# Mixing step of a spectral filter in front of a feed-forward network: scaled fp16 parts, moved to the end of odd slots, bias accumulated by TensorE, threshold read from PSUM

## Chip, cores and metric

One core of one Trainium2 chip. The metric is the device time of one execution in microseconds (us); the kernel before has 1456.93 us as the median of 3 runs (1455.4 to 1458.67).

## What is computed

```python
X = np.fft.rfft(x, axis=1)            # x: 4 batches, 3008 tokens, 256 features
Yr = Xr @ w_r - Xi @ w_i + b_r        # the mixing
Yi = Xr @ w_i + Xi @ w_r + b_i
Yr = sign(Yr) * max(abs(Yr) - 0.01, 0)   # the soft threshold, Yi alike
y = np.fft.irfft(Yr + 1j * Yi, n=3008, axis=1)
h = y @ w_in                          # 256 -> 2048
g = (a0 + a1*h + a2*h^2 + a3*h^3) / (1 + |b0|*|h| + |b1|*h^2 + 1e-6)
out = g @ w_out                       # 2048 -> 256
```

## The kernel before

The transform of 3008 = 64 x 47 points is split into matmul stages. **Stage 1** (`step_s1`, 64 groups g, fp32, 96 rows, 512 columns) transforms along 47; its result goes through DRAM. **Stage 2** (`step_s2`, 96 chunks c, 24 to a batch) transforms along 64; ScalarE takes its result out of PSUM into `xt` (`evacuate_s2`, L643, and a negated copy of one half, L644). **Stage 3** (`step_s3`, L438 and L439) is the mixing: four fp32 matmuls of 256 columns with `wr_sb` and `wi_sb` into one bank. VectorE adds the bias and -0.01 (`shifted`, L783, into `t1`), ScalarE makes the lower part of the threshold (`below`, L649), VectorE puts both together (`soft`, L789). **Stage 4** (`step_s4`, L445) is the first half of the inverse transform; `evacuate_s4` (L660) takes it out, and it is stored to DRAM. **Stage 5** (`step_s5`, L468) makes tiles of 470 tokens, which are split into two fp16 parts (L671, L857).

The **network** runs over 26 tiles t in 208 slots q, 8 to a tile. In a slot TensorE issues `group_f2_hi` (L506, L508) and `group_f2_lo` (L521) for slot q-3 and `group_f1` (L491, fp16 parts) for slot q+2. Around them ScalarE has five passes over 128x940 elements (L685, L688, L691, L751, L756), VectorE five (L911, L916, L891, L886, L897), and GpSimd the product `g_lo` (L967), which `group_f2_lo` waits for; a DMA from GpSimd's queue adds `sq` to `den` (L959).

The order of the work is written out by hand. The front (u = 0 to 30) has the first 29 chunks, 32 stage-1 groups, and the splitting of `w_in` and `w_out`. The other 67 chunks go into the slots: stage 2 at the end of an even slot q, stage 3 in slot q+1, stage 4 in slot q+3, both between `group_f2` and `group_f1` (L584 to L606). Stage-1 groups stand at the end of even slots of tiles 0 to 3 and 5 to 8 (`S1_SLOTS`, L114), stage 5 at the end of slots 1 and 3 of each tile 1 to 24 (`S5_AT`, L120). Stages 2, 4 and 5 share the PSUM bank `d0`, stages 1 and 3 the bank `d1`. A stage-5 step waits until every stage-4 result up to its own slot has been taken out of `d0`:

```python
if q and q in S2_AT or q in S5_AT:
    pe.wait_ge(e4, PRE + sum(1 for s in S2_AT if s + 3 <= q))
```

Each engine takes its instructions in order. ScalarE in iteration q: stage-2, stage-1 and stage-5 evacuations of slot q-1, `group(q+1)` with `below` inside it, a finished tile's output (L744, in slot 2 of a tile), L751 of q, `evacuate_s4`, L756 of q. VectorE in iteration q: L911, `shifted`, L916 of q, the stage-5 split, L891 of q-2, L886 of q-1, `soft`, L897 of q-2. `group_f1(q+2)` waits for L916 of q. GpSimd: L967 after L897, then L959. SyncE's queue issues all loads and stores of the transform.

Of the kernel before, what the change touches and what calls it, by code (L numbers as in the profile page):

```python
# [7 lines left out]
F32 = mybir.dt.float32  # L8
# [115 lines left out]
W_AT = 16  # L124
ENTRY = [t for t in range(2, NT) if len(tile_parts(t)) == 2]
# [40 lines left out]

def done_by(table, q, before):
    return before + sum(1 for s in table if s <= q)


def spectral_ffn(nc, x, c1, c5, fwd, inv, w_r, w_i, bias, w_in, w_out, coef_a, coef_b, out):
    with ExitStack() as ctx:
# [17 lines left out]
        wr_sb, wi_sb = sb("wr_sb", P, KH, D), sb("wi_sb", P, KH, D)  # L190
# [13 lines left out]
        qone, lam2 = sb("qone", P, 1), sb("lam2", P, 1)  # L204
# [8 lines left out]
        xt = several("xt", 2, P, KH, 192)  # L213
        t1, neg = sb("t1", P, D), sb("neg", P, D)
# [37 lines left out]
        STAGE = num + sq  # L252

# [26 lines left out]
        def _(sp):  # L280
# [137 lines left out]
        def _(pe):  # L418
# [16 lines left out]
            def step_s3(c, bank):  # L435
                pe.wait_ge(e2, (c + 1) * 2)
                for h in range(KH):
                    pe.matmul(bank[:, 0:D], xt[c % 2][:, h, 64:192], wr_sb[:, h, :], start=h == 0, stop=False)  # L438
                    mm = pe.matmul(bank[:, 0:D], xt[c % 2][:, h, 0:128], wi_sb[:, h, :], start=False, stop=h == 1)  # L439
                mm.then_inc(p3, 1)  # L440

            def step_s4(c, bank):
                pe.wait_ge(s_inv[c % 4], (c // 4 + 1) * 16)
                pe.wait_ge(m_thr, c + 1)
                pe.matmul(bank[:, 0:D], inv_in[c % 4][:, :], ythr[c % 2][:, :], start=True, stop=True).then_inc(p4, 1)  # L445

# [551 lines left out]
```

## Time and profile before

| | us |
|---|---|
| median of 3 runs | 1456.93 |
| the profiled execution, its own time | 1455.9 |
| its span in the profile | 1454.0 |
| TensorE matmul busy | 1411.5 (97%) |
| VectorE busy | 1261.2 (87%) |
| ScalarE busy | 1223.1 (84%) |
| GpSimd busy | 631.7 (43%) |

Busy shares are means over stages. Matmuls overlap in the records: the time that one takes is read from the start of one to the start of the next, or from the chain, which cuts them that way. An fp32 matmul has two records. The same holds on ScalarE and VectorE, where a record begins some 0.1 us before the one ahead of it has ended.

### The profile page before, as it was taken

How to read it: one execution, taken by the hardware profiler on the slowest of the kernel's cores; microseconds unless marked ns; L12 is line 12 of the kernel's file. 1: busy time of each engine (PE TensorE's matmuls, PEld its weight loads, DVE VectorE, ACT ScalarE, POOL GpSimd, SP SyncE). 2: the span in 40 equal slices, each digit the busy share in tenths (PEclk: the TensorE clock that was granted, in tenths of full speed). 3: DMA queues.
4: the chain of work that ended last, by engine and by line, in shares of the span. 5: the costliest groups of instructions: out<-in, count | busy, mean ns of one | idle time of the engine just before them, and what ended most of it. 6: DMA issues, size and time to landing. Idle time of an engine off the chain costs nothing.

```text
span 1454.0 us, 20392 instructions
## 1 busy us (share of the span) xinstructions
PE 1411.5 (97%) x7008; PEld 1004.7 (69%) x7008; DVE 1261.2 (87%) x1466; ACT 1223.1 (84%) x1687; POOL 631.7 (43%) x417
## 2 busy tenths in 40 slices
PE   7998999999999999999999999999999999999987
PEld 2886777777777777777777777776766666666666
DVE  0355988988988889889899989989989999999998
ACT  3567888988988888889878888888988999999986
POOL 0000444444444444445445545444545555555554
PEclk9999999999999999999999999999999999999999
DMA  9875666566466655655555555555554555555443
GB/s 276 246 249 140 144 156 135 134 143 145 100 138 140 144 117 130 142 103 124 110 120 112 122 110 118 120 110 106 116 115 100 100 105 111 115 113 105 89 96 70
DMA packets 97845, 188.00 MB, mean 129 GB/s; under 512 B 11152, under 2 KB 57680, under 8 KB 97744
## 3 DMA queue, kind: packets, MB, share of 16 engines
q0 software_dynamic: 29952, 98.58, 37.1%
q1 hardware_dynamic: 67792, 88.12, 20.6%
q8 instruction: 58, 0.95, 0.3%
q14 instruction: 43, 0.35, 0.1%
HBM read 50.60 MB, written 37.49 MB: 61 GB/s over the span
## 4 chain that ended last, share of the span: by engine, by line
PE 70%; DVE 17%; issue 5%; ACT 5%; DMA 2%; POOL 1%; SPq 0%; ACTq 0%; DVEq 0%; POOLq 0%
PE h_ps L491 23%; PE o_ps L521 8%; PE o_ps L506 8%; PE o_ps L508 8%; DVE den L891 4%; DVE num L897 4%; DVE g_hi L886 4%; PE d L439 4%; PE d L438 4%; DVE num L911 4%; PE d L468 3%; PE d L445 3%; PE d L431 2%; PE d L425 2%; PE h_ps L438 2%
## 5 line engine op out<-in xcount | busy, mean ns | idle before, releaser
L967 POOL TENSOR_TENSOR g_lo<-num,sq 128x940 fp32r<-128x940 f32 (+1 forms) x205 | 457.4, 2231 | 127.4 <-DVE num L897 127.2
L959 POOL DMA_DIRECT2D den<-sq x208 | 182.8, 879 | 682.4 <-PE o_ps L521 380.3
L506 PE MATMUL o_ps<-g_hi,wout_hi 128*128 128x470 f32 (+1 forms) x832 | 345.0, 415 | 0.9 <-DVE g_hi L886 0.9
L508 PE MATMUL o_ps<-g_hi,wout_lo 128*128 128x470 f32 (+1 forms) x832 | 310.3, 374 | 0.0
L491 PE MATMUL h_ps<-yt_hi,win_hi 128*128 128x470 f16 (+1 forms) x832 | 301.5, 362 | 3.9 <-DVE num L916 3.9
L491 PE MATMUL h_ps<-yt_lo,win_hi 128*128 128x470 f16 (+1 forms) x832 | 300.0, 361 | 0.0
L491 PE MATMUL h_ps<-yt_hi,win_lo 128*128 128x470 f16 (+1 forms) x832 | 299.6, 360 | 0.0
L685 ACT ACTIVATE den<-h_ps,coef 128x940 f32<-128x940 f32 (+1 forms) x208 | 214.2, 1030 | 53.1 <-PE h_ps L491 49.8
L916 DVE SCALAR_TENSOR_TENSOR num<-num,coef,h_ps 128x940 f32<-128x940 f32 (+1 forms) x208 | 244.5, 1175 | 5.0
L521 PE MATMUL o_ps<-g_lo,wout_hi 128*128 128x470 f32 (+1 forms) x832 | 225.9, 393 | 21.4 <-POOL g_lo L967 20.7
L897 DVE SCALAR_TENSOR_TENSOR num<-num,a_sb,den 128x940 f32<-128x940 f32 (+1 forms) x208 | 244.8, 1177 | 0.1
L886 DVE SCALAR_TENSOR_TENSOR g_hi<-num,a_sb,sq 128x940 fp32r<-128x940 f32 (+1 forms) x208 | 244.6, 1176 | 0.0
L911 DVE TENSOR_TENSOR num<-h_ps,num 128x940 f32<-128x940 f32 (+1 forms) x208 | 232.0, 1116 | 11.2 <-ACT num L691 11.0
L891 DVE SCALAR_TENSOR_TENSOR den<-den,g_hi 128x940 f32<-128x940 f32 (+1 forms) x208 | 237.1, 1140 | 0.1
L691 ACT ACTIVATE num<-h_ps,coef 128x940 f32<-128x940 f32 (+1 forms) x208 | 234.2, 1126 | 0.0
L688 ACT ACTIVATE sq<-h_ps,coef 128x940 f32<-128x940 f32 (+1 forms) x208 | 215.0, 1034 | 22.2 <-POOL g_lo L967 21.7
L751 ACT ACTIVATE sq<-den,qone 128x940 f32<-128x940 f32 (+1 forms) x208 | 223.4, 1074 | 3.2 <-DMA den<-sq 3.0
L756 ACT ACTIVATE sq<-sq 128x940 f32<-128x940 f32 (+1 forms) x208 | 204.2, 982 | 4.5
L521 PEld LDWEIGHTS o_ps<-g_lo,wout_hi 128*128 128x128 f32 x832 | 151.2, 189 | 58.8 <-POOL g_lo L967 40.4
L506 PEld LDWEIGHTS o_ps<-g_hi,wout_hi 128*128 128x128 f32 x832 | 158.0, 190 | 33.9 <-issue 8.3
L508 PEld LDWEIGHTS o_ps<-g_hi,wout_lo 128*128 128x128 f32 x832 | 158.1, 190 | 23.5 <-issue 7.4
L491 PEld LDWEIGHTS h_ps<-yt_hi,win_hi 128*128 128x128 f16 x832 | 81.4, 98 | 99.9 <-issue 33.3
(101 smaller groups left out, 1405.0 us busy)
## 6 DMA issues: line engine op xcount, KB each, us to landing
den<-sq POOLq DMA_DIRECT2D x200, 470.0 KB, 4.4
spec<-s1w SPq DMA_DIRECT2D x64, 192.0 KB, 3.2
z_in<-spec SPq DMA_DIRECT2D x96, 128.0 KB, 3.3
spec<-s_out SPq DMA_DIRECT2D x96, 128.0 KB, 3.3
xw<-in_x SPq DMA_DIRECT2D x31, 384.0 KB, 4.5
out_t<-o_sb SPq DMA_DIRECT2D x25, 470.0 KB, 4.7
zp_in<-spec SPq DMA_DIRECT2D x22, 480.0 KB, 4.8
inv_in<-in_inv SPq DMA_DIRECT2D x96, 64.0 KB, 2.4
```

What stands on the lines that cost most here:

```text
L491: mm = pe.matmul(h_ps[q % 2][:, j, 0:cols(q)], w[:, h, f * P:(f + 1) * P], y[t % 2][:, h, 0:cols(q)], start=i == 0, stop=i == len(terms) - 1)
L506: pe.matmul(o_ps[:, h, 0:w], wout_hi[:, f, h * P:(h + 1) * P], g_hi[q % 3][:, j, 0:w], start=f == 0, stop=False)
L508: mm = pe.matmul(o_ps[:, h, 0:w], wout_lo[:, f, h * P:(h + 1) * P], g_hi[q % 3][:, j, 0:w], start=False, stop=False)
L521: mm = pe.matmul(o_ps[:, h, 0:w], wout_hi[:, f, h * P:(h + 1) * P], g_lo[q % 2][:, j, 0:w], start=False, stop=f == FB - 1)
L691: act.activation(ring(num, q), h, ACT.Identity, bias=scales(q // SLOTS, 4), scale=scales(q // SLOTS, 5)).then_inc(n_num, 1)
L751: act.activation(ring(sq, q), ring(den, q), ACT.Abs_reciprocal_sqrt, bias=qone[:, 0:1]).then_inc(n_rs, 1)
L886: dve.scalar_tensor_tensor(out=g_hi[r % 3][:, :, 0:w], in0=ring(num, r), scalar=a_sb[:, 0:1], in1=ring(sq, r), op0=ALU.add, op1=ALU.mult). ...
L891: dve.scalar_tensor_tensor(out=ring(den, r), in0=ring(den, r), scalar=1.0 + 1e-6, in1=g_hi[r % 3][:, :, 0:cols(r)].bitcast(F32), op0=ALU.a ...
L897: dve.scalar_tensor_tensor(out=ring(num, r), in0=ring(num, r), scalar=a_sb[:, 0:1], in1=ring(den, r), op0=ALU.add, op1=ALU.subtract).then_ ...
L911: dve.tensor_tensor(top, h, top, ALU.mult).then_inc(n_n2, 1)
L916: dve.scalar_tensor_tensor(out=top, in0=top, scalar=scales(q // SLOTS, 1), in1=h, op0=ALU.add, op1=ALU.mult).then_inc(n_n3, 1)
L967: pool.tensor_tensor(g_lo[r % 2][:, :, 0:cols(r)], ring(num, r), ring(sq, r), ALU.mult).then_inc(n_g, 1)
```

## The change

It stores `w_r` and `w_i` as two scaled fp16 parts each (scale from their largest value), measures every batch of `x` by the sums of its absolute values, and scales the stage-2 result by that into fp16: ScalarE writes the upper part, VectorE the lower part and the negated halves. The mixing becomes one matmul that puts bias times scale into the bank and twelve fp16 matmuls. `shifted` and `t1` go; `below` and `soft` read the bank. The scale is taken out in `evacuate_s4`. Stages 4 and 3 move behind `group_f1`, `evacuate_s4` behind L756. The loads of `w_r`, `w_i` and the bias move up in SyncE's queue, into the stage-1 loop.

```diff
 # SyncE
             def load_x(k):
                 if k >= 4:
                     sp.wait_ge(p1, 2 * (k - 3))
+                    if k - 3 <= FRONT_S1 // 2:
+                        sp.wait_ge(x_dve, 2 * (k - 3))
+                    else:
+                        sp.wait_ge(x_act, 2 * (k - 3) - FRONT_S1)
...
+                if g == 8:
+                    load(mix_stage(0), w_r.rearrange("(h p) e -> p h e", p=P), s_wc)
+                    load(mix_stage(1), w_i.rearrange("(h p) e -> p h e", p=P), s_wc)
+                    load(bias_sb[:, :], bias, s_wc)
             load_fwd(0)
-            load(wr_sb[:, :, :], w_r.rearrange("(h p) e -> p h e", p=P), s_wc)
-            load(wi_sb[:, :, :], w_i.rearrange("(h p) e -> p h e", p=P), s_wc)
-            load(bias_sb[:, :], bias, s_wc)
 # TensorE
             def step_s3(c, bank):
-                pe.wait_ge(e2, (c + 1) * 2)
+                upper, lower = xt[c % 2][:, 0], xt[c % 2][:, 1]
+                pe.wait_ge(k_bias, 6)
+                pe.wait_ge(k_x, X_STEPS * (c // K2 + 1))
+                pe.matmul(bank[:, 0:D], picks[c // K2][:, :], bias_rows[:, :], start=True, stop=False)
+                pe.wait_ge(e2l, c + 1)
                 for h in range(KH):
-                    pe.matmul(bank[:, 0:D], xt[c % 2][:, h, 64:192], wr_sb[:, h, :], start=h == 0, stop=False)
-                    mm = pe.matmul(bank[:, 0:D], xt[c % 2][:, h, 0:128], wi_sb[:, h, :], start=False, stop=h == 1)
+                    pe.matmul(bank[:, 0:D], upper[:, h, 64:192], wr_hi[:, h, :], start=False, stop=False)
+                    pe.matmul(bank[:, 0:D], upper[:, h, 64:192], wr_lo[:, h, :], start=False, stop=False)
+                    pe.matmul(bank[:, 0:D], lower[:, h, 64:192], wr_hi[:, h, :], start=False, stop=False)
+                pe.wait_ge(e2n, c + 1)
+                for h in range(KH):
+                    pe.matmul(bank[:, 0:D], upper[:, h, 0:128], wi_hi[:, h, :], start=False, stop=False)
+                    pe.matmul(bank[:, 0:D], upper[:, h, 0:128], wi_lo[:, h, :], start=False, stop=False)
+                    mm = pe.matmul(bank[:, 0:D], lower[:, h, 0:128], wi_hi[:, h, :], start=False, stop=h == KH - 1)
                 mm.then_inc(p3, 1)
...
                 for r in done:
                     group_f2_hi(r)
-                if q - 3 in S2_AT:
-                    step_s4(c, d0[:, :])
                 for r in done:
                     if r < NS - 2:
                         group_f2_lo(r)
+                if q + 2 < NS:
+                    group_f1(q + 2)
+                if q - 3 in S2_AT:
+                    step_s4(c, d0[:, :])
                 if q - 1 in S2_AT:
-                    pe.wait_ge(m_t, c)
+                    pe.wait_ge(m_thr, c)
                     step_s3(c, d1[:, :])
-                if q + 2 < NS:
-                    group_f1(q + 2)
 # ScalarE
-                act.activation(xt[c % 2][:, :, 64:192], both, ACT.Copy).then_inc(e2, 1)
-                act.activation(xt[c % 2][:, :, 0:64], both[:, :, 64:128], ACT.Copy, scale=-1.0).then_inc(e2, 1)
+                act.wait_ge(k_x, X_STEPS * (c // K2 + 1))
+                act.activation(xt[c % 2][:, 0, :, 64:192], both, ACT.Identity,
+                               scale=x_scale[:, c // K2:c // K2 + 1]).then_inc(e2, 1)
+            def sum_abs(g):
+                act.activation(x_size[0:ROWS, :], x_in[...], ACT.Abs,
+                               accum_out=x_sum[0:ROWS, g:g + 1]).then_inc(x_act, 1)
...
                     act.activation(ring(sq, q), ring(den, q), ACT.Abs_reciprocal_sqrt, bias=qone[:, 0:1]).then_inc(n_rs, 1)
-                if q - 3 in S2_AT:
-                    evacuate_s4(S2_AT[q - 3], d0[:, :])
                 if q < NS:
                     act.wait_ge(n_rs, q + 1)
                     act.activation(ring(sq, q), ring(sq, q), ACT.Square).then_inc(n_rec, 1)
+                if q - 3 in S2_AT:
+                    evacuate_s4(S2_AT[q - 3], d0[:, :])
+                if q in S1_AT:
+                    sum_abs(S1_AT[q])
 # VectorE
+            def lower_x(c, bank):
+                dve.wait_ge(e2, c + 1)
+                dve.scalar_tensor_tensor(out=xt[c % 2][:, 1, :, 64:192], in0=both, scalar=x_scale[...],
+                                         in1=xt[c % 2][:, 0, :, 64:192], op0=ALU.mult, op1=ALU.subtract).then_inc(e2l, 1)
+                dve.wait_ge(e2l, c + 1)
+                dve.tensor_scalar(xt[c % 2][:, :, :, 0:64], xt[c % 2][:, :, :, 128:192], -1.0, None, ALU.mult).then_inc(e2n, 1)
...
-                if q - 2 in S2_AT:
-                    shifted(S2_AT[q - 2], d1[:, :])
                 if q < NS:
                     (L916)
+                if q - 1 in S2_AT and q >= 2:
+                    lower_x(S2_AT[q - 1], d0[:, :])
```

Added besides, in words: `sum_abs` of the 32 stage-1 groups of the front on VectorE (a `tensor_reduce` of 96x512 elements, one per group); at the start on VectorE the bias rows, the largest of `w_r` and `w_i`, six small steps for their scale and two subtractions for their lower parts, on ScalarE their upper parts; `measure_x(n)`, nine small dependent VectorE steps for each batch n, at the start, at u = 20, and in iterations 34 and 76, each behind a small matmul of TensorE (`sum_x`). The first stage-2 evacuation waits for `measure_x(0)`.

## Rows read from the trace of the kernel before

**Rows 1.** Busy time by stretch (busy us and count per engine, clock, DMA share, GB/s).
```profile
34.00:126.00 92.00, 91.80 (x459) 75.62 (x460) 41.83 (x118) 53.52 (x164) 0.00 (x0) 0.99 0.77 232
146.00:400.00 254.00, 253.72 (x1261) 183.88 (x1259) 224.06 (x249) 219.20 (x308) 114.64 (x75) 1.00 0.62 137
...
700.00:1000.00 300.00, 298.06 (x1512) 216.88 (x1513) 277.80 (x323) 260.85 (x353) 141.76 (x92) 1.00 0.55 117
1000.00:1300.00 300.00, 290.16 (x1440) 197.19 (x1438) 290.03 (x294) 271.12 (x308) 156.32 (x102) 0.99 0.53 108
```

**Rows 2.** Chain that ended last, slots 1 to 5 of a tile without stage 1 (start, us, what).
```profile
863.64 1.09 PE d L468 x10
...
869.71 0.44 PE d L431 x4
...
871.89 0.43 PE d L445 x2
872.32 0.94 PE o_ps L521 x4
873.26 0.43 PE d L438 x2
873.70 0.43 PE d L439 x2
...
874.99 2.38 PE h_ps L491 x12
```

**Rows 3.** Groups by line and shape, TensorE.
```profile
L508 PE MATMUL o_ps<-g_hi,wout_lo 128*128 128x470 f32 x800 | 300.6, 376 | 0.0
L491 PEld LDWEIGHTS h_ps<-yt_lo,win_hi 128*128 128x128 f16 x832 | 82.0, 99 | 69.5 <-issue 1.0
L438 PEld LDWEIGHTS d<-wr_sb,xt 128*128 128x128 f32 x268 | 50.8, 190 | 7.0
```

**Rows 4.** Groups by line and shape, ScalarE and VectorE.
```profile
L649 ACT ACTIVATE neg<-t,lam 128x256 f32<-128x256 f32 x96 | 48.6, 506 | 3.8 <-DVE t L783 3.8
L783 DVE TENSOR_TENSOR t<-d,bias_sb 128x256 f32<-128x256 f32 x67 | 27.9, 417 | 1.2
L643 ACT ACTIVATE xt<-d 128x256 f32<-128x256 f32 x67 | 25.2, 376 | 0.0
L644 ACT ACTIVATE xt<-d 128x128 f32<-128x128 f32 x67 | 18.2, 272 | 0.0
L636 ACT ACTIVATE s1w<-d 96x512 f32<-96x512 f32 x32 | 19.0, 595 | 4.9 <-PE d L425 4.9
L795 DVE TENSOR_REDUCE w_top<-num 128x1 f32<-128x1024 f32 x4 | 4.8, 1209 | 0.0
L698 ACT ACTIVATE win_hi<-num,w_scale 128x1024 f16<-128x1024 f32 x4 | 4.5, 1134 | 0.0
L700 ACT ACTIVATE wout_hi<-sq 128x1024 fp32r<-128x1024 f32 x4 | 4.2, 1045 | 0.0
L834 DVE TENSOR_SCALAR coef<-y_rec 128x1 f32<-128x1 f32 x7 | 1.1, 154 | 0.2
L865 DVE TENSOR_SCALAR minus_one<-ident 128x128 f16<-128x128 f32 x1 | 0.2, 217 | 0.0
```

**Rows 5.** Timeline of ScalarE, slots 2 and 3 of a tile with stage 1.
```profile
534.81 0.99 ACT L756 ACTIVATE sq<-sq 128x940 f32<-128x940 f32 x1
535.70 0.36 ACT L643 ACTIVATE xt<-d 128x256 f32<-128x256 f32 x1
...
540.71 1.00 ACT L756 ACTIVATE sq<-sq 128x940 f32<-128x940 f32 x1
543.46 0.65 ACT L671 ACTIVATE yt_hi<-d,coef 128x470 f16<-128x470 f32 x1 [1.75 <-PE d L468]
```

**Rows 6.** Timelines of GpSimd and VectorE, slots 4 and 5 of the tile of rows 2.
```profile
869.86 2.22 POOL L967 TENSOR_TENSOR g_lo<-num,sq 128x940 fp32r<-128x940 f32 x1 [1.14 <-DVE num L897]
...
870.85 1.19 DVE L916 SCALAR_TENSOR_TENSOR num<-num,coef,h_ps 128x940 f32<-128x940 f32 x1
```

**Rows 7.** Timeline of the start.
```profile
25.32 0.45 SPq L282 DMA_DIRECT2D wr_sb<-in_w_r  x1
...
31.40 0.29 DVE L777 TENSOR_SCALAR bias_sb<-bias_sb 128x256 f32<-128x256 f32 x1 [24.90 <-DMA bias_sb<-in_bias]
...
33.09 0.38 ACT L643 ACTIVATE xt<-h_ps 128x256 f32<-128x256 f32 x1 [4.38 <-PE h_ps L431]
```

More of the change, by code:

```diff
@@ L659, in evacuate_s4 @@
                     act.wait_ge(s_st4[c % 2], c // 2 * 16)
-                act.activation(s4_out[c % 2][:, :], bank[:, 0:D], ACT.Copy).then_inc(e4, 1)
+                act.activation(s4_out[c % 2][:, :], bank[:, 0:D], ACT.Identity,
+                               scale=x_inv[:, c // K2:c // K2 + 1]).then_inc(e4, 1)
             def evacuate_s5(idx, bank):
@@ L776, in _ @@
+            for g in range(FIRST_SUMS):
+                sum_abs(g)
             dve.wait_ge(s_wc, 16 * 3)
             dve.tensor_scalar(bias_sb[:, :], bias_sb[:, :], LAM, None, ALU.subtract).then_inc(k_dve, 1)
-            dve.wait_ge(k_dve, 9)
-            def shifted(c, bank):
-                dve.wait_ge(p3, c + 1)
-                dve.wait_ge(m_thr, c)
-                dve.tensor_tensor(t1[:, :], bank[:, 0:D], bias_sb[:, :], ALU.add).then_inc(m_t, 1)
-            def soft(c):
+            dve.wait_ge(k_dve, 8)
@@ new lines, in _ @@
+            dve.tensor_scalar(bias_rows[:, :], bias_sb[:, :], 1.0, None, ALU.mult).then_inc(k_bias, 1)
+            dve.memset(pick[:, :], 0.0).then_inc(k_bias, 1)
+            dve.wait_ge(k_bias, 2)
+            for half in range(2):
+                lo = half * 64 + 32
+                dve.scalar_tensor_tensor(out=bias_rows[lo:lo + 32, :], in0=bias_sb[lo:lo + 32, :], scalar=1.0,
+                                         in1=bias_rows[lo:lo + 32, :].bitcast(F32),
+                                         op0=ALU.mult, op1=ALU.subtract).then_inc(k_bias, 1)
+                dve.memset(pick[half * 64:half * 64 + 64, half * 64:half * 64 + 64], 1.0 / 32).then_inc(k_bias, 1)
@@ new lines, in _, with measure_x @@
+            dve.wait_ge(k_mix, 6)
+            for g in range(FIRST_SUMS, S1N + 4):
+                sum_abs(g)
+            def measure_x(n, part):
+                one, before = slice(n, n + 1), X_STEPS * n
+                dve.wait_ge(x_tot, n + 1)
+                dve.tensor_reduce(x_top[:, one], part, mybir.AxisListType.X, ALU.add).then_inc(k_x, 1)
+                dve.wait_ge(k_x, before + 1)
+                dve.tensor_scalar(x_top[:, one], x_top[:, one], 2.0 ** -50, None, ALU.max).then_inc(k_x, 1)
+                dve.wait_ge(k_x, before + 2)
+                dve.tensor_scalar(x_binade[:, one].bitcast(I32), x_top[:, one].bitcast(I32), 0x7F800000, None,
+                                  ALU.bitwise_and).then_inc(k_x, 1)
+                dve.wait_ge(k_x, before + 3)
+                dve.reciprocal(x_rec[:, one], x_binade[:, one]).then_inc(k_x, 1)
+                dve.tensor_scalar(x_inv[:, one], x_binade[:, one], 2.0 ** -3, mix_k[:, 0:1], ALU.mult, ALU.mult).then_inc(k_x, 1)
+                dve.wait_ge(k_x, before + 4)
+                dve.tensor_scalar(x_scale[:, one], x_rec[:, one], 2.0 ** 3, None, ALU.mult).then_inc(k_x, 1)
+                dve.tensor_scalar(x_out[:, one], x_rec[:, one], 2.0 ** 3, mix_scale[:, 0:1], ALU.mult, ALU.mult).then_inc(k_x, 1)
+                dve.wait_ge(k_x, before + 7)
+                dve.tensor_scalar(x_lam[:, one], x_out[:, one], -2.0 * LAM, None, ALU.mult).then_inc(k_x, 1)
+                dve.tensor_scalar(picks[n][:, :], pick[:, :], x_out[:, one], None, ALU.mult).then_inc(k_x, 1)
+                dve.wait_ge(k_x, before + X_STEPS)
@@ L859, in split_lo @@
                                          op0=ALU.mult, op1=ALU.subtract).then_inc(e5l, 1)
+            for i, (part_hi, part_lo) in enumerate(((wr_hi, wr_lo), (wi_hi, wi_lo))):
+                dve.wait_ge(mix_hi, i + 1)
+                dve.scalar_tensor_tensor(out=part_lo[:, :, :], in0=mix_stage(i), scalar=mix_scale[:, 0:1],
+                                         in1=part_hi[:, :, :], op0=ALU.mult, op1=ALU.subtract).then_inc(mix_lo, 1)
+            measure_x(0, d1[:, 0:S1N])
+            lower_x(0, h_ps[0][:, 0, :])
             for u in range(1, PRE + 1):
-                shifted(u - 1, h_ps[1][:, (u - 1) % 2, :])
+                if u < PRE:
+                    lower_x(u, h_ps[0][:, u % 2, :])
                 if u == W_AT + 11:
```

165 lines of the change are left out of this document (130 added, 35 removed).

## The prediction
> **What bounds the kernel now.** I read the busy times by stretch first, then the chain, then the timelines around the moved steps. In the front (34 to 126 us) and in the slots with spectral work (146 to about 1000) TensorE has next to no idle time: 91.80 of 92.00, 253.72 of 254.00 and 298.06 of 300.00 us [rows 1]. Behind it VectorE is at 224 of 254 and 278 of 300, ScalarE at 219 and 261. From 1000 on VectorE is the full one (290.03 of 300) with TensorE at 290.16; there the 96 mixing steps are nearly all done. So columns taken from TensorE are time up to about 1000 us, as long as the order of the work doesn't turn them into waits.
>
> **The mixing on TensorE.** Today: four fp32 matmuls, 0.43 us apart and 1.73 in all (873.26 to 874.99) [rows 2]. After: twelve fp16 matmuls of 256 columns. A record of stage 2 is also 256 column cycles (128 columns, two passes), and four of them take 0.44, 0.11 each [rows 2]; a stretch of twelve with 470 fp16 columns takes 2.38, 0.198 each, 0.42 ns per column, so 256 give 0.108. Twelve are 1.30. The bias matmul by L508's pace (0.214 for 470, eight in the 1.73 of a group) is 0.12. Sum 1.42, saving 0.31 a step: 67 x 0.31 = 20.8 us in the slots and 29 x 0.31 = 9.0 in the front, **29.8 together**. Bounds for one step: 1.35 below, 1.6 above (a change between number formats costs up to 0.1, twice).
> Whether the weight loads stay hidden decides this. An fp16 load has a record of 99 ns, an fp32 load 190 [rows 3], and stage 2 hides the longer one behind the same 256 cycles, so I take them as hidden. The Trainium skill, TensorE: Matmul & The Clock Gate, The mechanism, says that a load overlaps matmuls in flight only when its row group differs, which here it never does. By that rule a pair would take 0.108 + 0.099 = 0.21, a step 2.6 us, and the sum would be 80 us slower instead. By that rule the 2.38 us of twelve fp16 matmuls would be impossible too, so the trace speaks against it.
>
> **VectorE.** Out goes L783 (0.42, net 0.34), in come the lower part (by L783's form about 0.4) and the negation of 256 fp16 elements (by L865's 217 ns for 128, and at most 0.4) [rows 4]: +0.3 a chunk, four chunks a tile, 1.2 us on a tile's 53 to 56 us, against the 7 to 12% that it is idle [rows 1]. It stays covered as long as TensorE bounds; over the last 20 chunks, where VectorE is at 93% and more, it may cost up to 3 us, 0 taken. The lower part waits for the stage-2 evacuation, which ends about 536.1 [rows 5], some 5 us ahead of stage 3's new place. The Trainium skill, SBUF — State Buffer, Who interferes with whom, says that a `tensor_scalar` in a two-port mode and a GpSimd operation lock each other out for a whole instruction. By it the negation could wait for `g_lo`. `g_lo` ends at 872.08, L916 in front of the lower part at about 871.96 [rows 6], so the lower part passes the remainder and the sum would not change by more than 0.2 us a chunk in front of an engine with slack.
>
> **ScalarE.** L644 goes (net 0.15), an Identity with a scale costs 0.09 over a Copy (L698 against L700), twice, and each stage-1 group in the slots gets `sum_abs`: L636's 0.59 + 0.13 (L649's accumulating form against L643's) + 0.09 to read the sum - 0.1 overlap = 0.7 [rows 4]. `below` waits for stage 3 itself, no longer for VectorE: it comes 1.9 us behind `group_f1`, just what two passes ahead of it take, so 0.
>
> **What the new order turns into waits.**
> (a) Stage 5 in slot 3 needs the stage-4 result of its own slot out of the bank. Today that result came before `group_f1`; now 1.4 us before stage 5, and its evacuation stands behind L756. With stage 1 in the tile: L756 starts at 540.71 [rows 5]; -0.15 + 0.09 + 0.70 ahead of it, -0.27 for the evacuation that leaves, +0.13 for the semaphore that it covered, gives 541.21, +0.89 for the pass, +0.36 for the evacuation, +0.1: stage 5 can start at 542.55. TensorE would be there at 543.46 - 0.20 - 1.09 - 0.31 = 541.86. Loss 0.7 in 7 tiles: **4.9**. In the 10 tiles without stage 1 ScalarE is 1.2 earlier and TensorE 0.85: nothing left to wait for.
> (b) `group_f2_lo` loses stage 4's cover. In slot 5 GpSimd ends at 872.08 [rows 6], the group begins at 872.32 + (0.94 - 0.86) = 872.40 [rows 2], and would now be due at 871.89: 0.5 of wait against 0.08 today. Loss 0.43 in the 10 tiles without stage 1 (with it, 0.85 us more lie ahead): **4.3**. Slot 1 of these tiles is half as tight: **2.0** (0 to 4.3).
> (c) `measure_x` of two batches in iterations 34 and 76 stands in front of L897, nine dependent steps at L834's 0.154 and more, 1.5 us, and by `g_lo` it reaches `group_f2_lo`: **3.0** (0 to 4).
> (d) Front: where the network's weights are split (8 of 29 steps) ScalarE's round (0.36 + 0.49 + 0.36 + 1.05 and waits) is as long as TensorE's new 2.3, and `measure_x(1)` falls there; the DMA share is already 0.77: **3.5** of the 9.0 (1 to 8).
> (e) Start: today L643 begins at 33.09, and the weights' loads are issued at 25.3 behind the stores [rows 7]. They move to about 15 us, three issues of 0.45 and 640 KB in front of stores; on VectorE follow bias rows (2 us), two maxima (0.65 each by L795), eight sums of stage-1 input (0.65), two lower parts (0.65), `measure_x(0)` 1.7; I get the first stage-2 evacuation at about 35 instead of 33.1, and add the stores' delay: **3.0** (0 to 7).
> The moved stage 4 makes its store some 4 us later; what is queued behind it on SyncE (z, inverse matrices, stage-1 stores, the next tile's input) is issued more than a slot ahead of its use, the tightest at the batch borders in slots 39 and 87. Taken as 0; if the slack is gone, 2 to 4 us at two places. `shifted`'s place, the renumbered waits at the start and `lower_x` at q = 0 cost nothing: TensorE has `group_f1(0)` over them.
>
> **Sum.** 29.8 - 4.9 - 4.3 - 2.0 - 3.0 - 3.5 - 3.0 = 9.1 us less than the profiled execution's 1455.9, 1446.8; the median of the runs is 1.0 above that execution, so **1448**.
>
> **Rivals.**
> A, the columns come through nearly whole: the waits (a) and (b) are covered by slack that I don't see, since ScalarE begins its passes 1.9 us earlier relative to the slot's end. For it: 1.75 us of idle ScalarE before L671 [rows 5]. Against it: that idle time is counted in (a). Time: 1457 - 29.8 + 6 = 1433; chance 0.16.
> B, slower: in the slots with stage 5 ScalarE becomes the bound. Its place is the wait on `e4` in front of L468, its price 1 us a tile for each us that ScalarE gets later, in all 17 tiles with chunks. It decides from 0.6 us beyond my sum on (9.1 over 17). `sum_abs` or the fp16 evacuation priced too low, or L751 waiting for its DMA once ScalarE runs earlier, would do it; at 1.2 us beyond it 20 us are lost: 1459, at 1.5 some 1464. For it: VectorE and GpSimd hang on the same iterations. Against: every pass has its row. Chance 0.14.
> C, weight loads not hidden (above), 1535: 0.02.
> D, the gain is spent in full but no more: start and front at their upper bounds (7 and 8): 1456.5, 0.10.
> E, the change doesn't do what it says, as the pace of an fp16 matmul with 256 columns is 0.13: nothing is saved, 1457 + 6 = 1463, 0.04.
> My forecast (gain of 3 to 16) has 0.54.
>
> **Numbers.** What a measurement can tell from no change is about 0.2%, 2.9 us. Faster by more: 0.54 + 0.16 = 0.70 (all of forecast and A), within 0.12, slower 0.18 (B, C, E and the upper end of D). The range reaches from 1434 (A) to 1461 (most of B, all of D); outside are C and E, the far end of A and of B.
>
> **What would show it.** Stage-3 steps of 1.4 us in the chain, twelve records 0.108 apart; waits of some 0.7 us in front of L468 in slot 3 of tiles with stage 1, released by the stage-4 evacuation; waits for `g_lo` in odd slots; TensorE idle some 2% in 146 to 1000 where it had none; a tile with stage 1 shorter by about 0.5 us. Wrong would be: a pace over 0.12; the stage-5 wait over 1 us in all tiles; a front that is no shorter; or stretches from 1000 on that change.

## The result, and the profile after

The changed kernel takes 1453.92 us (median of 20 runs, 1451.39 to 1456.76), the kernel before, run beside it, 1457.84 (20 runs). The ratio of the two is 0.9977, 95% interval 0.997 to 0.9984: **3.9 us by the medians, 0.23% by the ratio, faster**. That is inside the range (1434 to 1461), with 3.9 us gained where 9 were forecast. The profiled execution has a span of 1451.9 us against 1454.0.

The head of the page of the changed kernel (busy us, share, count):

```profile
span 1451.9 us, 21569 instructions
...
PE 1394.3 (96%) x7498; PEld 972.0 (67%) x7498; DVE 1319.5 (91%) x1645; ACT 1253.8 (86%) x1657; POOL 630.4 (43%) x417
```

TensorE's busy time fell by 17 us, the span by 2. VectorE's rose by 58 (some of it the sums of `x` in the front). The stretches, to be laid beside [rows 1]:

```profile
34.00:126.00 92.00, 88.90 (x632) 71.73 (x632) 57.87 (x172) 58.31 (x142) 0.30 (x1) 0.99 0.79 236
146.00:400.00 254.00, 250.72 (x1362) 177.05 (x1361) 231.03 (x287) 230.18 (x317) 114.01 (x75) 1.00 0.62 138
400.00:700.00 300.00, 294.86 (x1600) 207.38 (x1599) 272.59 (x334) 268.37 (x368) 132.89 (x88) 1.00 0.57 127
700.00:1000.00 300.00, 294.87 (x1614) 208.37 (x1612) 283.89 (x343) 264.11 (x331) 141.37 (x92) 0.99 0.54 117
```

TensorE now has gaps everywhere: 3.3 us of 254, 5.1 of 300 and 5.1 of 300, where it had 0.3, 0.5 and 1.9. The mixing step in the chain (start, us, what), to be laid beside [rows 2]:

```profile
858.92 0.43 PE d L486 x2
859.36 0.12 PE d L470
859.47 0.12 PE d L473
859.60 0.11 PE d L474
...
860.69 0.11 PE d L480
860.80 1.10 PE d L522 x10
```

From 859.36 to 860.80 it takes 1.44 us, where it took 1.73. That is what was predicted for the mixing; the loss is elsewhere. The new and changed instructions by form (busy us, mean ns, idle before and its releaser), against [rows 3, 4]:

```profile
L743 ACT ACTIVATE s_out<-d,x_inv 128x256 f32<-128x256 f32 x96 | 45.0, 468 | 11.1 <-PE d L486 5.0 <-DMA spec<-s_out 3.9 <-PE d L511 1.2
L931 DVE SCALAR_TENSOR_TENSOR xt<-d,x_scale,xt 128x256 f16<-128x256 f32 x67 | 32.2, 480 | 10.7 <-ACT xt L715 10.7
L934 DVE TENSOR_SCALAR xt<-xt 128x256 f16<-128x256 f16 x96 | 21.8, 227 | 3.3
L723 ACT ACTIVATE x_size<-xw 96x512 f32<-96x512 f32 x32 | 19.7, 615 | 0.0
L475 PEld LDWEIGHTS d<-wr_hi,xt 128*128 128x128 f16 x134 | 13.1, 98 | 1.5
```

And who keeps TensorE waiting between 146 and 1000 us (waits: us in total, times, longest):

```profile
PEld o_ps L575 <- POOL g_lo L1134: 17.6, 22, 2.5
PE o_ps L575 <- POOL g_lo L1134: 9.9, 18, 2.1
PEld d L522 <- ACT s_out L743: 6.1, 8, 1.0
PE d L522 <- ACT s_out L743: 3.8, 8, 0.6
```

L575 is `group_f2_lo`, L522 stage 5. These are the two waits (a) and (b) of the prediction. (The waits of PE and of its weight loads PEld overlap and are not to be added.) Of the 9.9 us in front of L575, 5.5 are three waits that (b) does not have: 1.65 and 1.70 behind the two measurements, 2.12 at a batch border.

**Tile by tile.** The loop was measured tile by tile, from the start of VectorE's first pass (L911, now L1073) in one tile's first slot to that in the next tile's. Length of a tile in us:

| tile (first slot) | before | after | change | predicted |
|---|---|---|---|---|
| stage 1, four chunks (16, 24, 48, 56, 64; mean) | 55.79 | 55.42 | -0.37 | -0.54 |
| the same, batch border (40) | 55.82 | 56.25 | +0.43 | -0.54 |
| four chunks, `measure_x` (32, 72; mean) | 53.51 | 55.17 | +1.66 | +0.9 |
| four chunks (80, 104, 120; mean) | 52.94 | 52.26 | -0.68 | -0.6 |
| four chunks, batch border (88) | 54.40 | 56.14 | +1.74 | -0.6 |
| three chunks (96, 112, 128; mean) | 50.60 | 51.13 | +0.53 | -0.3 |

(The predicted column divides the prediction's own terms: 0.31 a chunk, less 0.7, less 0.43 + 0.2, or plus 1.5.) Two tiles of the loop are not in the table: tile 8 went from 55.79 to 55.64, tile 136, the last with mixing steps, from 55.94 to 54.06. From slot 8 to slot 144 all adds up to 918.5 us before and 919.7 after. All that the kernel gained it gained ahead of slot 8 (4.4 us there, 3.2 at slot 144, 2.0 at slot 152 and from there on); tiles 136 and 144 together have -0.7 (-1.88 and +1.21).

### The profile page after: what moved, and what is told of

The parts are those of the page before. It is cut to its first block, busy times and chain, and to the rows that moved or that the text cites. A ratio compares the mean times of both kernels' runs of the same rounds, so it can differ in the third digit from the quotient of the medians.

```text
span 1451.9 us, 21569 instructions
## 1 busy us (share of the span) xinstructions
PE 1394.3 (96%) x7498; PEld 972.0 (67%) x7498; DVE 1319.5 (91%) x1645; ACT 1253.8 (86%) x1657; POOL 630.4 (43%) x417
## 3 DMA queue, kind: packets, MB, share of 16 engines
HBM read 50.60 MB, written 37.49 MB: 61 GB/s over the span
## 4 chain that ended last, share of the span: by engine, by line
PE 53%; DVE 22%; ACT 11%; issue 7%; POOL 4%; DMA 2%; SPq 0%; ACTq 0%; DVEq 0%; POOLq 0%
PE h_ps L545 18%; PE o_ps L575 7%; DVE den L1053 5%; DVE num L1059 5%; PE o_ps L560 5%; DVE g_hi L1048 5%; PE o_ps L562 5%; POOL g_lo L1134 4%; DVE num L1073 3%; PE d L522 3%; PE d L486 2%; ACT num L775 2%; ACT sq L772 2%; ACT den L769 2%; ACT sq L839 2%
## 5 line engine op out<-in xcount | busy, mean ns | idle before, releaser
L1134 POOL TENSOR_TENSOR g_lo<-num,sq 128x940 fp32r<-128x940 f32 (+1 forms) x205 | 452.1, 2205 | 176.6 <-DVE num L1059 176.0
L560 PE MATMUL o_ps<-g_hi,wout_hi 128*128 128x470 f32 (+1 forms) x832 | 341.1, 411 | 2.2 <-DVE g_hi L1048 2.2
L575 PE MATMUL o_ps<-g_lo,wout_hi 128*128 128x470 f32 (+1 forms) x832 | 216.7, 382 | 31.4 <-POOL g_lo L1134 30.7
L1073 DVE TENSOR_TENSOR num<-h_ps,num 128x940 f32<-128x940 f32 (+1 forms) x208 | 231.8, 1115 | 8.1 <-ACT num L775 7.8
L839 ACT ACTIVATE sq<-den,qone 128x940 f32<-128x940 f32 (+1 forms) x208 | 223.4, 1074 | 3.3 <-DMA den<-sq 3.3
L575 PEld LDWEIGHTS o_ps<-g_lo,wout_hi 128*128 128x128 f32 x832 | 150.6, 189 | 74.0 <-POOL g_lo L1134 55.7
```

The costliest lines, as they stand in the source:

```text
L560: pe.matmul(o_ps[:, h, 0:w], wout_hi[:, f, h * P:(h + 1) * P], g_hi[q % 3][:, j, 0:w], start=f == 0, stop=False)
L575: mm = pe.matmul(o_ps[:, h, 0:w], wout_hi[:, f, h * P:(h + 1) * P], g_lo[q % 2][:, j, 0:w], start=False, stop=f == FB - 1)
L839: act.activation(ring(sq, q), ring(den, q), ACT.Abs_reciprocal_sqrt, bias=qone[:, 0:1]).then_inc(n_rs, 1)
L1073: dve.tensor_tensor(top, h, top, ALU.mult).then_inc(n_n2, 1)
L1134: pool.tensor_tensor(g_lo[r % 2][:, :, 0:cols(r)], ring(num, r), ring(sq, r), ALU.mult).then_inc(n_g, 1)
```

## The experiments

All times are medians beside runs of the kernel before on the same chip (1456.9 to 1457.6 there). Tiles are named by their first slot. The diffs are against the changed kernel, except for the first.

Two limits hold for all of them. The changed kernel was not run again beside them, and the kernel before moved by up to 0.9 us between the sets (1456.94 to 1457.84), so a difference from the changed kernel is good to about 1 us. And one execution of each kernel is profiled: its first stage-2 matmul begins at 33.56 us in the changed kernel and at 33.89 to 36.24 in its variants, also where the edit is only in the slots. So what an edit does in the slots is read from the lengths of the tiles, and the medians say it only roughly.

### The new order alone

The order of the change in the kernel before, arithmetic as it was (TensorE's part is shown; the stage-4 evacuation also goes behind L756):

```diff
+                if q + 2 < NS:
+                    group_f1(q + 2)
                 if q - 3 in S2_AT:
...
                     step_s4(c, d0[:, :])
...
                 if q - 1 in S2_AT:
...
                     step_s3(c, d1[:, :])
-                if q + 2 < NS:
-                    group_f1(q + 2)
```

> The kernel before with the new order alone: stages 4 and 3 behind group_f1, the stage-4 evacuation behind L756; mixing in fp32, bias and threshold as before. Theory O (the order turns cover into waits: group_f2_lo for g_lo, stage 5 for the stage-4 evacuation): slower than before by 4 to 9 us, with waits of some 0.4 us in front of group_f2_lo in odd slots of the tiles without stage 1. Theory V (the added work on VectorE takes the gain, the order costs nothing): within 2 us of before.

Measured: 1481.86 us, ratio 1.0168 (1.0153 to 1.0182), 24 us slower than before, far more than either theory had. The trace names a wait that had none before (VectorE's waits, 146 to 1000 us):

```profile
DVE t L783 <- PE d L439: 97.1, 59, 3.1
```

`shifted` stands ahead of L916 on VectorE, and stage 3 now comes behind `group_f1`, so VectorE stands still for it, 1.6 us a chunk; a part of that was idle time before. The order is only usable once `shifted` is gone. The two halves of the change belong together, and the order alone is no gain.

### The new arithmetic in the old order

TensorE's part is shown; the stage-4 evacuation also goes back ahead of the Square.

```diff
-                for r in done:
-                    if r < NS - 2:
-                        group_f2_lo(r)
-                if q + 2 < NS:
-                    group_f1(q + 2)
                 if q - 3 in S2_AT:
...
                     step_s4(c, d0[:, :])
+                for r in done:
+                    if r < NS - 2:
+                        group_f2_lo(r)
...
                     step_s3(c, d1[:, :])
+                if q + 2 < NS:
+                    group_f1(q + 2)
```

> The changed arithmetic in the order of before: stage 4 between group_f2_hi and group_f2_lo, stage 3 between group_f2_lo and group_f1, the stage-4 evacuation ahead of L756. If the order alone is what costs (theory O with nothing to force the order), it is 5 to 9 us faster than the changed kernel. If the order is forced, because VectorE now reads the stage-2 result after L916 of the same slot and stage 4 needs that bank, TensorE waits about 1 us in front of stage 4 in each of 67 odd slots: slower than the changed kernel by 20 us or more, the waits released by the line of lower_x.

Measured: 1460.44, ratio 1.0016 (1.0007 to 1.0026): 6.5 us slower than the changed kernel, and slightly slower than before too, so neither forecast of the expectation was met. (One of its 11 executions took 5870.77 us, for which nothing on record gives a reason; the median does not hang on it.) TensorE's waits (146 to 1000 us):

```profile
PE d L486 <- issue: 19.3, 24, 2.3
```

Stage 4 stands ahead of `group_f1` and waits there, in 24 slots and not in 67; its releaser is not in the records, so that it is `lower_x` is not shown. By tiles, 3.3 us of the 6.5 lie behind slot 8, 1.6 in tile 0 and 1.7 in a later start. It takes the new order to make the cheaper mixing pay.

### TensorE relieved by four more matmuls a step

The four matmuls with `lower` are left out, and so is the part of the product that they carry:

```diff
-                    pe.matmul(bank[:, 0:D], lower[:, h, 64:192], wr_hi[:, h, :], start=False, stop=False)
...
-                    mm = pe.matmul(bank[:, 0:D], lower[:, h, 0:128], wi_hi[:, h, :], start=False, stop=h == KH - 1)
```

> The changed kernel without the four matmuls a chunk that take the lower part of the stage-2 result (so that part of the product is left out); VectorE still computes it. TensorE has 0.44 us less in 96 chunks, 42 us. If TensorE bounds front and slots alike, it is 35 to 42 us faster than the changed kernel. If the other engines are level with it in the slots (theory V), the front gives its 12 us and the slots at most half of their 29: 15 to 27 us faster.

Measured: 1436.53, ratio 0.9852 (0.9834 to 0.987). 96 steps x 4 x 0.108 = 42 us were taken from TensorE, and 17 came through. The front (first stage-2 matmul to first `group_f1`) took 86.4 us, with the change 86.2: there TensorE's columns no longer set the time. The total lies in the second forecast (15 to 27), its parts do not: the front, which was to give its 12 us, gave none, and slots 8 to 144 gave 17.8. In the slots a tile with stage 1 went from 55.42 to 54.12, 1.30 of the 1.73 us of matmuls that left it, a four-chunk tile without stage 1 from 52.26 to 51.50, 0.76 of 1.73. Cut into pairs of slots, tile 104 reads 12.08, 14.27, 13.84, 12.09 us with the change and 12.08, 13.49, 13.84, 12.08 here: only the second pair is shorter. The first and the last did not move although TensorE had 0.43 us less to do in them. That pointed to VectorE, and the last experiment takes it up.

### The stage-4 evacuation back ahead of the Square

```diff
+                if q - 3 in S2_AT:
+                    evacuate_s4(S2_AT[q - 3], d0[:, :])
                 if q < NS:
                     act.wait_ge(n_rs, q + 1)
                     act.activation(ring(sq, q), ring(sq, q), ACT.Square).then_inc(n_rec, 1)
-                if q - 3 in S2_AT:
-                    evacuate_s4(S2_AT[q - 3], d0[:, :])
```

> The changed kernel with the stage-4 evacuation put back ahead of L756. ScalarE passes it some 0.9 us earlier, but in the slots before stage 5 it must then wait for stage 4, which now ends late. If stage 5's wait for it is worth what the prediction says (0.7 us in 7 tiles), 2 to 5 us faster; if ScalarE stands in front of it waiting for stage 4 and passes that on to VectorE by L756, no gain or a loss of up to 5 us.

Measured: 1450.42, ratio 0.9948 (0.9935 to 0.996), 3.5 us less than the changed kernel. The wait is that of term (a). ScalarE in the changed kernel, in the slots of [rows 5]:

```profile
535.66 1.08 ACT L839 ACTIVATE sq<-den,qone 128x940 f32<-128x940 f32 x1
536.78 0.99 ACT L842 ACTIVATE sq<-sq 128x940 f32<-128x940 f32 x1
537.67 0.46 ACT L743 ACTIVATE s_out<-d,x_inv 128x256 f32<-128x256 f32 x1
539.57 0.65 ACT L755 ACTIVATE yt_hi<-d,coef 128x470 f16<-128x470 f32 x1 [1.44 <-PE d L522]
```

Stage 5 (L522) cannot begin before L743 has ended at 538.13. With the two passes exchanged it begins 0.97 us behind the start of L839 (534.03, 535.00 there), and not 2.01. One tile of each kernel (changed first, then with the passes exchanged), busy us per engine:

```profile
507.35:562.76 55.41, 54.97 (x298) 38.62 (x297) 49.51 (x59) 50.45 (x72) 24.62 (x17) 1.00 0.59 133
```

```profile
505.81:560.55 54.74, 54.74 (x298) 38.62 (x296) 49.65 (x59) 50.13 (x72) 24.64 (x16) 1.00 0.60 134
```

The seven tiles with stage 1 and stage 5 are shorter by 0.66 to 0.91 each, 5.1 together, where (a) had 0.7 and 4.9; four-chunk tiles without stage 1 are as long as they were (52.23), also as (a) had it. The median shows less of it (3.5); in the profiled execution the start and tile 0 are 2.4 us later (slot 8 at 176.38 for 174.03). Of the eight waits of stage 5 one is left in TensorE's list:

```profile
PE d L522 <- ACT s_out L743: 0.6, 1, 0.6
```

### The measurement of x: left out, and moved

`one_scale` scales batches 2 and 3 by the measure of batch 1 and leaves theirs out; `x_hidden` does them ahead of the stage-5 split instead of behind `soft` (the diff is of its VectorE part; a wait is added in front of `below` on ScalarE):

```diff
+                for n in (2, 3):
+                    if q == X_AT[n] + 1:
+                        measure_x(n, d1[:, D:D + S1N])
                 if q - 1 in S5_AT and S5_AT[q - 1] // KH not in LATE_TILES:
                     split_lo(S5_AT[q - 1], d0[:, :])
...
-                for n in (2, 3):
-                    if q == X_AT[n] + 1:
-                        measure_x(n, d1[:, D:D + S1N])
```

> The changed kernel without measure_x for batches 2 and 3 (left out: they use the scale of batch 1); the sums of absolute values stay. The two tiles with a measurement took 55.17 us in the changed kernel where their neighbours of the same kind take 52.2 to 52.5. If the measurement on VectorE is what they pay, both lose 2 to 2.5 us: 4 to 5 us faster than the changed kernel (the prediction's term was 3.0). If VectorE had slack there, under 1 us.

Measured: 1449.00, ratio 0.994 (0.9926 to 0.9953). Tiles 32 and 72 went from 55.17 to 53.49 and 53.48. So a measurement costs 1.7 us; on VectorE it stands for 1.5 (360.96 to 362.43), which is what term (c) had. The forecast of 2 to 2.5 a tile was not met: the median's 4.9 us are 3.4 in the two tiles, and the rest is in no tile of the loop.

> The changed kernel with measure_x of batches 2 and 3 ahead of the stage-5 split of the same iteration, where VectorE idles 2 to 2.7 us waiting for stage 5, instead of between L1048 and L1059. Nothing is left out. If its place on the way to g_lo is what costs, the gain is that of one_scale, 4 to 5 us. If the work itself costs wherever it stands, no gain.

Measured: 1450.48, ratio 0.9949 (0.9936 to 0.9961). The two tiles take 53.81 and 53.80: moved by a few lines, the nine steps cost 0.3 instead of 1.7. Ahead of the split VectorE waits anyway, for stage 5 and ScalarE; behind `soft` it is `g_lo` that is late, and TensorE with it: its waits of 1.65 and 1.70 us in slots 35 and 77 are gone. The two tiles make 2.7 us. The profiled execution has besides 1.7 less in tile 88 and 1.2 in tile 144, where nothing was moved; both are TensorE's clock, below.

### The coefficients of a new batch, two iterations later

```diff
-                        if SETS[i][-1] == n:
+                        if SETS[i][-1] == n and not (n < B - 1 and SETS[i] == (n,)):
                             coefficients(i)
...
+                for n in range(1, B - 1):
+                    if q - 3 == Y_AT[n]:
+                        coefficients(SETS.index((n,)))
```

> The changed kernel with the second set of coefficients at the two batch borders (nine small steps of VectorE, 1.25 us) two iterations later, in the idle time ahead of the stage-5 split. If TensorE's waits there (2.12 us for g_lo, and a stretch of 3.4 us at half clock behind the second one) come from VectorE's queue, 2 to 4.5 us faster than the changed kernel, with no half-clock stretch near 740 us. If the half clock has another cause, at most 2.4 us faster and the stretch stays.

Measured: 1448.95, ratio 0.9938 (0.9926 to 0.9951). Tile 40 went from 56.25 to 55.04, tile 88 from 56.14 to 53.35, and tile 144, where nothing was moved, from 46.35 to 45.10. What stands there with the change (VectorE's timeline, iteration 88; 18 small steps in a row, the first and last two shown, and the passes behind them):

```profile
727.83 0.18 DVE L967 TENSOR_REDUCE y_top<-d 128x1 f32<-128x24 f32 x1
728.04 0.21 DVE L969 TENSOR_SCALAR y_top<-y_top,x_inv 128x1 f32<-128x1 f32 x1
...
730.50 0.28 DVE L988 TENSOR_SCALAR coef<-a_sb,y_k 128x2 f32<-128x2 f32 x1
730.82 0.21 DVE L990 TENSOR_SCALAR coef<-coef,y_k 128x1 f32<-128x1 f32 x1
731.07 1.14 DVE L1053 SCALAR_TENSOR_TENSOR den<-den,g_hi 128x940 f32<-128x940 f32 x1
```

From 727.83 to 731.07 VectorE does 3.2 us of these; the run moves the last seven (729.87 to 731.07, 1.2 us; its expectation says nine). They were there before as well (L969 without its factor), and then cost tile 88 some 1.5 us (54.40 against 52.94). With the change they cost 3.9.

Some 1.7 of that is TensorE's clock. TensorE waits for `g_lo` behind that border, and `group_f1` comes next (TensorE's timeline of the changed kernel, then two stretches of it, whose columns are those of [rows 1]):

```profile
737.09 1.12 PE L575 MATMUL o_ps<-g_lo,wout_hi 128*128 128x470 f32 x4 [2.12 <-POOL g_lo L1134]
...
738.66 0.60 PE L545 MATMUL h_ps<-yt_hi,win_lo 128*128 128x470 f16 x1
739.06 0.60 PE L545 MATMUL h_ps<-yt_hi,win_hi 128*128 128x470 f16 x1
```

```profile
732.00:737.00 5.00, 2.97 (x17) 2.15 (x14) 4.96 (x8) 1.97 (x3) 2.14 (x1) 1.00 0.63 138
738.00:742.30 4.30, 4.30 (x14) 1.93 (x14) 4.26 (x5) 3.09 (x4) 2.12 (x2) 0.60 0.56 104
```

The granted clock was 0.60 in the second stretch, most of it at 1.2 GHz, and the matmuls of `group_f1` begin 0.39 us apart instead of 0.2. With the coefficients put off, TensorE's wait in the same place was 0.94 us and no slow stretch followed. But the length of the wait does not decide it. In `x_hidden`, whose edit is not in this tile, the wait is as long and the clock stays:

```profile
735.34 1.12 PE L575 MATMUL o_ps<-g_lo,wout_hi 128*128 128x470 f32 x4 [2.11 <-POOL g_lo L1136]
```

```profile
730.25:735.25 5.00, 2.98 (x17) 2.15 (x14) 4.96 (x8) 1.99 (x3) 2.13 (x1) 1.00 0.55 112
736.25:740.55 4.30, 4.30 (x28) 2.85 (x28) 4.26 (x5) 3.52 (x5) 2.11 (x2) 1.00 0.56 104
```

Tile 88 takes 54.45 us there, 1.7 less than with the change. So the border run shows 1.2 us in tile 40 and 1.1 in tile 88 for the coefficients; that it also prevents the slow stretch is not shown.

### VectorE's negation: given to GpSimd, and left out

```diff
-                dve.wait_ge(e2l, c + 1)
-                dve.tensor_scalar(xt[c % 2][:, :, :, 0:64], xt[c % 2][:, :, :, 128:192], -1.0, None, ALU.mult).then_inc(e2n, 1)
+                if c <= PRE:
+                    (both lines)
...
+                    pool.wait_ge(e2l, c + 1)
+                    pool.wait_ge(e2n, c)
+                    pool.tensor_scalar(xt[c % 2][:, :, :, 0:64], xt[c % 2][:, :, :, 128:192], -1.0, None, ALU.mult).then_inc(e2n, 1)
```

> The changed kernel with the negation of the 66 chunks in the slots on GpSimd, behind its DMA issue. VectorE has 0.2 us less in every odd iteration. If VectorE bounds the pairs of slots without stage 5 (12.08 us in every kernel, even with a third of the mixing left out), they go to about 11.88, and the kernel is 3 to 7 us faster than the changed one. If TensorE is the bound, no change; if GpSimd's queue gets late (its step stands in front of the next g_lo), slower.

Measured: 1454.80, ratio 0.9975 (0.9966 to 0.9985), no different from the changed kernel. In tiles with stage 1 the first pair of slots fell from 12.90 to 12.80 us and the last rose from 12.08 to 12.37. GpSimd takes 1.16 to 1.19 us for what VectorE does in 0.23, and has the next `g_lo` behind it; that this is what takes the saving back is argued, not shown.

The other run has no negation in the slots at all (it leaves those halves stale):

> The changed kernel without the negation on VectorE for the 66 chunks in the slots (the negated halves are left as they were: that part of the product is left out). TensorE's work is the same; VectorE has 0.2 us less a chunk. Where TensorE bounds (tiles with stage 1, 55.42 us) nothing moves. Where VectorE is the last releaser, its 0.2 us comes through: the tiles with three chunks (12, 14 and 16 at 51.14, 50.70 and 51.55) lose 0.4 to 0.6 each, tiles with four chunks and no stage 1 (52.28) 0.2 to 0.8. Sum 3 to 8 us faster than the changed kernel. If VectorE has slack everywhere, under 1 us.

Measured: 1451.45, ratio 0.9959 (0.9943 to 0.9975), 2.5 us less, of which tile 88 (no slow stretch there) has 1.9. In tile 104 the pairs of slots are 11.96, 14.65, 13.83, 11.82, the sum 52.26 as with the change. So VectorE's saving appears in the first and the last pair, and the second gives it back.

### TensorE and VectorE relieved together

Both of these left out (the four matmuls and the negation), no other edit:

> Leaves out the four fp16 matmuls with the lower part of x (as in no_lower, 1436.5 us) and VectorE's negation in the slots (as in no_neg, 1451.5 us), together. Theory 1, VectorE is the bound in the first and the last pair of slots of every tile with chunks: there VectorE has no wait at all and a pair takes 12.08 us with the change (11.68 before), 12.08 in no_lower too, though TensorE has 0.43 us less to do. Then both parts left out must give more than the two alone do: the last pair goes to 11.81, the first to 11.8 or 11.9, and since TensorE is no longer near, the middle pairs do not take it back: a tile of four chunks is shorter by 0.5 to 0.8 than in no_lower (51.50), 16 tiles, so 1425 to 1430 us. Theory 2, the middle pairs of a tile bound the loop through TensorE's waits for the remainder and for the stage-4 evacuation, and what VectorE saves at the ends of a tile is waited for in the middle, as in no_neg, whose tiles are as long as those of the changed kernel: a tile of four chunks stays at 51.4 to 51.6 and the run at 1434 to 1437.

Measured: 1432.43, ratio 0.9828 (0.9812 to 0.9845): 4.1 us less than with the four matmuls alone, between the two theories. Four-chunk tiles without stage 1 go from 51.50 to 50.97, three-chunk tiles by as much (50.72, 50.28, 50.78 to 50.18, 49.75, 50.25); the pairs of tile 104 are 11.81, 13.51, 13.84, 11.81. Stage-1 tiles stay at 54.1. Tile 88 has the slow stretch of the clock again (granted 0.65 and 0.50 from 724 to 728) and 55.14 us for 54.02, so without it the two would have given some 1 us more (an estimate from these two lengths). Theory 1 holds for the second half of the loop and theory 2 for tiles with stage 1. The last pair of a four-chunk tile, in the kernel before, with the change, and with TensorE relieved:

```profile
875.23:886.91 11.68, 11.68 (x60) 8.65 (x59) 11.64 (x15) 10.54 (x15) 6.15 (x4) 1.00 0.70 150
```

```profile
873.03:885.12 12.09, 12.09 (x68) 8.60 (x68) 11.98 (x16) 11.10 (x15) 6.15 (x4) 1.00 0.66 146
```

```profile
861.31:873.39 12.08, 12.07 (x65) 8.26 (x64) 11.97 (x15) 11.17 (x15) 6.19 (x4) 1.00 0.68 149
```

VectorE (third busy time) is full in all three, and has no wait in any. TensorE shows as full too, in the third with four matmuls less. Its records run past the next matmul's start (0.36 us each, begun 0.20 apart, in `group_f1`) and hide the slack. In this pair VectorE was full before the change already: 11.08, a pair of slots without mixing, plus 0.60 for `shifted` and `soft`. With the change it is 11.08 + 1.00.

### A better version

The exchanged evacuation, the measurement ahead of the split and the later coefficients, together; nothing is left out:

> The changed kernel with the three moves together: stage-4 evacuation ahead of L756, measure_x ahead of the stage-5 split, the second set of coefficients two iterations later. Nothing is left out. If the three losses are separate, their gains add: 3.5 + 3 + 4 = 10 to 11 us faster than the changed kernel, about 1443, 1.0% faster than the kernel before. If they share one slack, under 7.

Measured: 1441.89, ratio 0.9893 (0.9879 to 0.9907), 15 us less than before and 12 less than the change. The three gains of the medians add up (3.5 + 3.4 + 5.0), but in part by luck, since the slow stretch that is missing in tile 88 and 1.2 us of tile 144 stand in the profiles of both of the last two. By tile the profile has: tiles 32 and 72 -3.0, tile 40 -1.85, the other six with stage 1 and stage 5 -4.5, tile 88 -2.8, tile 144 -1.4, and tile 0 +0.5. Its stretches:

```profile
146.00:400.00 254.00, 253.46 (x1379) 179.61 (x1378) 234.54 (x290) 230.92 (x322) 115.28 (x76) 1.00 0.63 140
400.00:700.00 300.00, 299.06 (x1636) 212.34 (x1635) 277.26 (x341) 270.65 (x376) 135.15 (x89) 1.00 0.58 130
700.00:1000.00 300.00, 295.82 (x1624) 209.80 (x1622) 286.14 (x345) 262.89 (x333) 143.32 (x93) 1.00 0.55 117
```

TensorE's gaps in the first two are down from 3.3 and 5.1 us to 0.5 and 0.9. Past 700, with no stage 1 left, 4.2 of 5.1 remain.

> As best, with both sets of coefficients of a batch border put off, the first by two iterations and the second by four, each into the idle time ahead of a stage-5 split. If VectorE's queue is what TensorE waits for at the borders, another 1 to 2.4 us faster than best. If the first set is then late for the evacuation behind that stage 5, slower than best by up to 2 us.

Both sets of coefficients put off (2 and 4 iterations): 1442.10, ratio 0.9892 (0.9877 to 0.9907), the same. What a border still costs is not to be had this way.

## Why the prediction was right and wrong

**The mixing step** was right: 1.44 us for 1.42, matmuls 0.11 apart, loads hidden at a record of 98 ns. Rival C fell, and with it, for this kernel, the rule of the Trainium skill (TensorE: Matmul & The Clock Gate, The mechanism) that a load overlaps only when its row group differs; the same section also lets a load into the background weight buffer go ahead, which the prediction left out and this result does not contradict. Rival E fell too. The negation never ran beside `g_lo` (none of its 96 records begins inside one, the longest is 0.23 us), so whether the two shut each other out was not seen.

**The front** was right in size: from the first stage-2 matmul to the first `group_f1` 91.6 us became 86.2, -5.4 for the predicted 9.0 - 3.5. The start cost 1.7 in the profiled run and up to 4.4 in the experiments, for 3.0 (0 to 7). The run with four matmuls less says why the front gave back what it did: TensorE is not its bound any more.

**(a)** was right in place, size and tiles: 0.7 us, in stage-1 tiles only. **(b)** was right in place, with waits of 0.23 and 0.25 us in tile 104 for the 0.20 and 0.43 of the sum. That four-chunk tiles gained 0.68 for 0.6 is luck in part: in tile 104 the first three pairs of slots gained 1.04 and the last, which was to gain 0.31, lost 0.41. **(c)** was priced at 1.5 a measurement and cost 1.7; the tile without it (53.49) is no shorter than before (53.51) either, where 0.6 was to be gained. Why not was not tried.

**What failed is the step "VectorE: stays covered, 0 taken".** The +0.3 a chunk was +0.40 (1.00 for 0.60), a smaller error. The larger one was that I took TensorE's full busy time in a stretch of 300 us for the bound of every slot in it. VectorE, 93% busy over the stretch, was without a gap in the last pair of a tile without stage 1; its idle 7% lay in the other pairs, as its waits before show (146 to 1000 us; in tile 104 they stand in slots 104, 106 and 108):

```profile
DVE yt_lo L857 <- ACT yt_hi L671: 58.7, 29, 2.6
DVE ythr L789 <- ACT neg L649: 20.6, 22, 1.2
```

The last pair was to get shorter by 0.31 and got longer by 0.40. In four-chunk tiles the other pairs covered that (12.51 to 12.08, 14.55 to 14.27, 14.17 to 13.84). In three-chunk tiles they did not: +0.53 for -0.3, 2.5 us over three tiles, near the upper bound of 3 us that the prediction named for the last 20 chunks and then took as 0. In tile 96 it is the first pair too, 11.07 to 11.74: it had no mixing work on VectorE and now has a lower part with its negation, a fourth in a tile of three. That removing the negation shortens just these pairs is shown; that it accounts for the whole of the three tiles is not, since without it they shrink by 0.52, 0.23 and nothing.

The same step failed at **the batch borders**. I had looked there for a late store and not at VectorE's 3.2 us of coefficients, whose cover was TensorE's spare time: 1.0 us in tile 40 and 2.3 in tile 88 beyond the sum. Of the 3.3, 1.7 are the slow stretch of the clock, which came behind the wait here and did not behind the same wait in `x_hidden`: that part is chance as far as the record goes, and no step of the prediction. Moving the coefficients took 1.2 and 2.8 off the two tiles, the 1.7 among them.

Against the prediction the profiled execution misses 7.0 us: borders 3.3, three-chunk tiles 2.5, measurement tiles 1.5, stage-1 tiles 1.2, less 0.2 in four-chunk tiles, 0.7 ahead of slot 8 and 0.7 in tiles 136 and 144 (rounded). So the failed step makes 4.1 of it (2.5 and the 1.6 of the borders that are not clock), the clock 1.7. Tile 136 was to stay as it was and gained 1.88, for which no reason was looked for. **Rival A** had (a) and (b) covered; both are there. **Rival D** came near in its time (1456.5), not in its reason: the start and the front stayed below its bounds. **Rival B** named the wrong engine for the same kind of thing: an engine behind TensorE that becomes the bound. ScalarE, 264 of 300 us busy, did not. Its times were also added wrong: 20 us lost beyond a forecast of 1448 give 1468, not 1459, and 1.5 us a tile some 1474.

Unsettled: what holds the middle pairs of tiles with stage 1 (54.1 us with TensorE, or TensorE and VectorE, relieved), and the slow stretch of TensorE's clock near 1090 us, which the kernel before has too but shorter (granted clock from 1090 to 1100 us 0.83 before, 0.67 after), and where tile 144 lost 1.2 (46.35 for 45.14). Tile 144 is as short as before in the runs with the measurement, the coefficients or the negation moved, for which no reason was tested.

## What to carry to other kernels

Look for the bound in the smallest stretch that repeats, here two slots, and ask which engine has no wait in it; matmul records that fill a stretch don't make TensorE its bound. When the leading engine is relieved by x, every piece of work that another engine does once in a while (a measurement, new coefficients) loses up to x of its cover: price each with none, and put it where its engine waits anyway. A pass that frees a buffer for the next stage goes ahead of one that doesn't.

## What was unexpected of the hardware

TensorE's clock fell from 2.4 to 1.2 GHz in the middle of a nearly full loop, behind a single wait of 2.12 us (the stretch before it had 2.97 us of matmuls in 5), and made `group_f1` 4.08 us long instead of 2.40. So a wait can cost nearly its own length again. The wait alone does not bring it: `x_hidden` has 2.11 us in the same place, with 2.98 us of matmuls in the 5 us around it, and the run with four matmuls less 2.74, both at a granted clock of 1.00 behind it; one of 1.65 in tile 32 of the changed kernel had no slow stretch behind it either. In slot 143 TensorE waits 3.82 us before and 3.54 with the change, and the clock fell behind it in every kept profile but that of the run with both relieved. So a tile's length can differ by 1.7 us between two kernels whose difference lies elsewhere; what else decides was not tried.
